# Moving one k and q step ahead of a decay step, and pairing two more head pairs, in a linear-attention and two-MLP kernel

## The reference

```python
for t in range(S):                      # 768 tokens, state is 48 x 48 for each batch and head
    state = alpha[:, :, t, :, None] * state + einsum('bhd,bhe->bhde', k[:, :, t], v[:, :, t])
    y[:, :, t] = einsum('bhd,bhde->bhe', q[:, :, t], state)
x = y as (batch * token, head * 48)
x = square(maximum(x @ w_in, 0)) @ w_out          # first MLP
out = silu(x @ w2_in) @ w2_out                    # second MLP
```

## Time and profile before

| what | value |
|---|---|
| median of 3 runs | 886.68 us (886.6 to 889.64) |
| the profiled execution's own time | 888.62 us |
| its span on the core | 887.0 us |
| PE busy | 862.5 us, 97% of the span |
| DVE busy | 544.8 us, 61% |
| ACT busy | 436.5 us, 49% |
| mean granted PE clock over the span | 0.99 |

### The profile page before, as it was taken

One profiled execution on the slowest core, in us unless ns is written; L12 is line 12 of the kernel. 1 busy time (PEld: TensorE's weight loads), 2 busy tenths in 40 slices (PEclk: granted clock), 3 DMA queues, 4 the chain that ended last, 5 costly groups with the idle time before them and its releaser, 6 DMA issues.

```text
span 887.0 us, 17687 instructions
## 1 busy us (share of the span) xinstructions
PE 862.5 (97%) x6834; PEld 714.2 (81%) x6834; DVE 544.8 (61%) x1090; ACT 436.5 (49%) x788; POOL 106.1 (12%) x127
## 2 busy tenths in 40 slices
PE   7999999998999899989999999999999999999998
PEld 6778788887778777878888888888888888888898
DVE  7789888877576657653234565555855446766620
ACT  5756654454445445534567654445543336545510
POOL 3463200000000000000165003002020003000000
PEclk9999999999999899989999999999999999999999
DMA  8884444334242414100321353000130000110010
GB/s 169 232 235 110 107 114 113 79 84 106 55 107 71 97 31 101 55 18 11 116 72 54 66 113 89 1 1 1 37 107 0 1 1 1 36 37 1 1 48 28
DMA packets 134204, 60.04 MB, mean 68 GB/s; under 512 B 81824, under 2 KB 129312, under 8 KB 134112
## 3 DMA queue, kind: packets, MB, share of 16 engines
q1 hardware_dynamic: 130800, 58.14, 26.6%
q10 hardware_dynamic: 3312, 0.69, 0.4%
HBM read 45.02 MB, written 9.44 MB: 61 GB/s over the span
## 4 chain that ended last, share of the span: by engine, by line
PE 83%; DVE 8%; issue 4%; ACT 3%; SPq 1%; DMA 1%; DVEq 0%; ACTq 0%
PE h_ps L1239 20%; PE z_ps L1210 17%; PE h_ps L1196 17%; PE z_ps L1275 11%; PE jobs L1275 7%; PE jobs L1295 3%; DVE decay L1784 3%; DVE decay L1769 2%; DVE kp L1738 2%; PE jobs L1062 1%; PE jobs L1073 1%; PE h_ps L1295 1%; ACT g L1507 1%; ACT g L1513 1%; DVE kp L1802 1%
## 5 line engine op out<-in xcount | busy, mean ns | idle before, releaser
L1507 ACT ACTIVATE g<-h_ps 128x512 f32<-128x512 f32 x96 | 57.1, 595 | 170.0 <-PE h_ps L1196 167.9
L1899 DVE TENSOR_TENSOR g_lo<-g,g_hi 128x512 fp32r<-128x512 f32 x96 | 68.1, 712 | 101.9 <-ACT g L1513 101.8
L1601 ACT ACTIVATE sum<-sum 128x512 f32<-128x512 f32 x96 | 60.6, 631 | 137.2 <-DVE sum L1960 112.2
L1960 DVE TENSOR_TENSOR sum<-h_ps,sum 128x512 f32<-128x512 f32 x120 | 82.9, 691 | 56.5 <-PE h_ps L1239 53.9
L1196 PE MATMUL h_ps<-x_hi,win_hi 128*128 128x512 f32 x288 | 114.1, 396 | 2.5 <-DVE x_lo L1891 0.9
L1210 PE MATMUL z_ps<-g_hi,wout_hi 128*128 128x512 f32 x282 | 115.4, 409 | 0.0
L1196 PE MATMUL h_ps<-x_lo,win_hi 128*128 128x512 f32 x288 | 112.3, 390 | 0.0
L1196 PE MATMUL h_ps<-x_hi,win_lo 128*128 128x512 f32 x288 | 112.2, 390 | 0.0
L1210 PE MATMUL z_ps<-g_hi,wout_lo 128*128 128x512 f32 x282 | 112.2, 398 | 0.0
L1210 PE MATMUL z_ps<-g_lo,wout_hi 128*128 128x512 f32 x282 | 111.9, 397 | 0.0
L1239 PE MATMUL h_ps<-s_hi,t_hi 128*128 128x512 f32 x264 | 103.1, 390 | 0.2 <-DVE sum L1960 0.2
(11 more groups left out here) (185 smaller groups left out, 1597.4 us busy)
## 6 DMA issues: line engine op xcount, KB each, us to landing
z_scratch<-z_sb SPq DMA_DIRECT2D x18, 256.0 KB, 2.7
pre<-z_scratch SPq DMA_DIRECT2D x18, 256.0 KB, 3.8
v_sb<-in_v SPq DMA_DIRECT2D x44, 96.0 KB, 2.5
out_x<-z_stage SPq DMA_DIRECT2D x80, 48.0 KB, 1.7
nat_a<-in_alpha SPq DMA_DIRECT2D x40, 88.0 KB, 2.3
nat_k<-in_k SPq DMA_DIRECT2D x40, 88.0 KB, 2.2
nat_q<-in_q SPq DMA_DIRECT2D x40, 88.0 KB, 2.3
nat_a<-in_alpha SPq DMA_DIRECT2D x40, 80.0 KB, 2.2
```

The costliest lines, as they stand in the source:

```text
L1507: nc.scalar.activation(g[f % 2][:], h_ps[f % 2][:], ACT.Relu).then_inc(act_made, 1)
L1601: nc.scalar.activation(at[:], at[:], ACT.Silu).then_inc(silu_made, 1)
L1899: nc.vector.tensor_tensor(low, g[f % 2][:], high.bitcast(F32), ALU.subtract).then_inc(g_lo_made, 1)
L1960: nc.vector.tensor_tensor(to[:], h_ps[(PRODUCTS * n + r) % 2][:], other[:], ALU.add).then_inc(summed, 1)
```

## The change

For the couples that go by the formula, KQ of the first pair moves from base - 1 to base - 2, which is the step of the second pair's A. In DVE's order within a step KQ comes before A. Pairs 4 and 5 become a couple, with steps of their own in the table. Pair 5 then uses the output tile `y_sb[0]`, as every coupled pair does, and its scores go into `y_sb[1]`; three waits follow this.

```diff
 def coupled(n):
-    return n >= COUPLED
+    return n >= COUPLED or n // 2 == PAIRS // 2
...
     if first < 14:
-        at = {8: {"A": 13, "KQ": 14, "S": 16, "I": 19, "Y": 20}, 9: {"A": 16, "KQ": 17, "S": 19, "I": 20, "Y": 22},
+        at = {4: {"A": 1, "KQ": 2, "S": 4, "I": 7, "Y": 8}, 5: {"A": 4, "KQ": 6, "S": 7, "I": 8, "Y": 10},
+              8: {"A": 13, "KQ": 14, "S": 16, "I": 19, "Y": 20}, 9: {"A": 16, "KQ": 17, "S": 19, "I": 20, "Y": 22},
...
     if n % 2 == 0:
-        return base + {"A": -4, "KQ": -1, "S": 0, "I": 3, "Y": outputs}[kind]
+        return base + {"A": -4, "KQ": -2, "S": 0, "I": 3, "Y": outputs}[kind]
...
             def y_copy(n):
                 y_slot_free(n // PAIRS, n % PAIRS)
-                if n > COUPLED:
+                if n > PAIRS and coupled(n - 1):
                     wait(act, y_moved[(n + 1) % 2], moved((n + 1) // PAIRS, (n + 1) % PAIRS))
...
             def a_turn(n):
-                if coupled(n):
+                if n > PAIRS + 1:
                     wait(dve, kt_made, n - 1)
...
             def s_stage(n):
-                wait(dve, y_made, n - 1 if n > COUPLED else n)
-                if n == COUPLED + 1:
+                wait(dve, y_made, n - 1 if coupled(n) and coupled(n - 1) else n)
+                if n in (PAIRS + 1, COUPLED + 1):
                     wait(dve, y_moved[n % 2], moved(n // PAIRS, n % PAIRS))
```

## The result

The changed kernel takes 875.46 us (median of 4 runs, 874.21 to 876.59), against 888.02 us for the kernel before on the same chips (4 runs, 886.6 to 889.64). The ratio is 0.9858, 95% interval 0.9829 to 0.9886. The profiled execution took 874.47 us with a span of 872.8 us, so 14.2 us less than the 887.0 us of before; 14.6 us were forecast.

The account below looks back on a forecast made before the run. PE was taken as the bound, nearly always busy, idling 12.0 us at the scores of five pairs. Waits 6.9, clock 7.4 and pairs 4 and 5 0.3 sum to 14.6 us: 888.62 to 874.0 us, range 867.5 to 880.0.

Parts of the forecast that it names:

- The scores' wait goes: PE's wait at the scores, 12.0 us over five couples, disappears because q is ready at about 203.8.
- It moves to the next first product: First products wait for the addition of Y, held by the later decay through ACT's queue: 1.6 or 0.9 us each.
- The gain of a couple is 2.61 us less d: d is the decay's delay on DVE; gains of 1.44 us three times and 1.27 us twice, 6.9 us in sum.
- The clock's 7.4 us: PE's lower clock behind waits at the scores cost 7.4 us by twin stretches; all of it counted as won.
- the rival with the falling clock: The clock still falls behind the remaining waits, so 3 to 7 us stay lost: 877 to 881.4 us; chance 0.15.
- Pairs 4 and 5, 0.3 us: Making pairs 4 and 5 a couple wins 0.2 to 0.5 us net, taken as 0.3 us.
- the rival of the costly second part: DVE adds pair 4's outputs late behind pair 6's decay, costing 2 to 4 us at worst: 877 us; chance 0.06.
- The median: The median of the runs was taken as 874.0 us, or 872.1 if 1.9 us are a fixed part of profiling.
- The claim that the spread goes: The 3 us by which runs of the kernel before differ should go where all waits are short.
- The stall did not go altogether: Rival: the output copy is not held by the sum of squares, no stall remains: 867.7 us; chance 0.12.
- The slower outcome: Rival: k and q find no idle time on DVE, d is 3.49 us: 892.7 us; chance 0.03.

Follow-up runs that it names:

- kernel with d = 3.49 us: The changed kernel with k and q of the first pair behind the low part, still ahead of the second pair's decay: 894.09 us, ratio 1.0044.
- kernel that keeps PE busy: The kernel before with 14 matmuls of 128x256 on PE ahead of the scores of pairs 14, 16, 18, 20 and 22: 881.36 us, ratio 0.9908.
- the first part alone: The kernel before with k and q of the first pair at base - 2 for five couples, pairs 4 and 5 single: 876.0 us, ratio 0.9837.
- all waits: The later-sum-of-squares kernel with the first pair's decay at base - 5 (couples 16, 20) and pair 4's output copy ahead of two weight copies: 867.94 us.

## Why the prediction was right, point by point

**The scores' wait goes.** Right: no wait at L1063, in all five couples. q was ready at 202.97 + 0.69 = 203.66 (203.8 forecast).

**It moves to the next first product and is held by the decay through ACT's queue.** Right, and shown rather than argued: with the sum of squares behind the copy all five waits went. The forecast waits were 1.6 us three times and 0.9 us twice; 1.37, 1.33 and 1.02 us, and 0.57 and 0.59 us, were seen. The starts were forecast better than the idle times, since an idle time is counted from the modelled end of the last matmul: product 37 came 7.89 us behind product 36, and 213.75 - 205.83 = 7.92 us was forecast.

**The gain of a couple is 2.61 us less d.** Right. Gains are counted here from first product base to base + 2. In the couples whose stretch had run at full clock before, the changed kernel gained 1.35 us (pair 14) and 1.24 us (pair 20), for 1.44 and 1.27 forecast. The term was 0.09 us too large for pair 14, because a first product that waits makes its next step 0.13 us longer (4.21 us; 4.09 in the kernel before, where product 37 did not wait). Couple 22 did not quite follow the pattern of 14, as the prediction has it: its wait was 2.49 us before and is 1.02 us now. The kernel with d = 3.49 us confirms the other side: its waits are 2.2 to 2.4 us longer.

**The clock's 7.4 us.** Right. Couples 16, 18 and 22 gained 2.84, 4.27 and 4.32 us; less the gain of their twins (1.24, 1.35, 1.35) this is 1.60, 2.92 and 2.97 us, against 1.61, 2.91 and 2.91. The kernel that keeps PE busy gave 7.41 us by the clock alone. The Trainium skill's way of pricing it, in "TensorE: Matmul & The Clock Gate", section "Terms", gave an estimate of 8.1 us, which was 0.7 us too high. Part of a half-clock stretch does not double: the 32 score matmuls took 0.69 us at full clock and 1.13 us at half clock (granted clock 0.50 from 296.28 to 298.00), which is 1.6 times as long.

```profile
296.28 1.13 PE L1062 MATMUL jobs<-qp,kp 48*64 48x64 f32 x32 [2.84 <-issue]
```

Of the waits that remain (1.37 us at most) none brought the clock down, and in the ten runs with k and q moved (four of the changed kernel, six of the first part alone) the mean clock is 0.999 or 1.00, so the rival with the falling clock is out for this kernel. The prediction had two reasons for this: the waits are shorter, and they lie between large matmuls. The second does not hold by itself, since waits of 2.8 to 3.7 us at the same place brought the clock down four times in five. There is some luck in the size: 7.4 us is what one execution lost, and the kernel before lost more or less from run to run.

**Pairs 4 and 5, 0.3 us.** Nothing that can be told from zero: counted from first product 0, product 36 stood 0.09 us earlier in the changed kernel, and 0.31 us later in the one with this part alone. The wait of first product 9 was forecast at 0.3 us and was 0.43 us, but its cause as forecast (two weight copies on ACT) was wrong. It is the decay of pair 6, which the rival of the costly second part named, at a smaller price. That the wait was forecast at about its size, from the wrong operations, is luck.

**The median.** 874.0 was forecast and 875.46 measured. The claim that the spread goes holds for the part that the clock made. On one chip 23 runs of the kernel before took 884.37 us (mean clock 0.996) to 896.58 us (0.983), and 6 runs of the first part alone 874.27 to 876.56 us. A spread of 2 us remains, which the prediction had not seen (last section); runs at its longer end lift the median over the sum.

**The rivals.** The stall did not go altogether, since the copy is held as said. The slower outcome needs d above 2.61 us: the kernel with k and q behind the low part has it, and took 894.09 us, 3.2 us more than the kernel before on its chip (892.7 us, or 4.1 us more, forecast).

## What to carry to other kernels

Before a late operation is moved ahead of another, ask who waits for that other one, and on which engine's queue: here moving k and q won 1.2 to 1.4 us of waits of 1.9 to 2.8 us, beside what the clock gave, and the rest needed an operation moved on another engine. Price a move by the idle time that it fills, not by the wait that it removes; the same move behind one more operation, where it fills none, made the kernel slower. A wait of PE can cost more than its length, where the clock falls behind it; filling it with matmuls that do nothing tells that share apart.

## What the runs showed of the hardware

The lower clock followed waits unevenly. In the kernel before it fell at the waits ahead of pairs 16, 18 and 22 (1.94, 2.84 and 2.49 us), and not at those of 14 and 20 (2.84 and 1.94 us). In the kernel with pairs 4 and 5 alone, whose waits are the same to 0.02 us, it fell at 14, 18 and 22. So the same wait of 2.84 us brought it in one execution and not in the other. Of waits of 2.8 to 3.7 us for the addition of Y four in five did, and none of the waits of first products of 1.4 us or less. The fall need not come at once: at pair 16 the clock was still 1.00 from 253.20 to 254.80, over the small matmuls behind the wait, and 0.50 from 255 to 257. The kernel before took from 884.37 to 896.58 us on one chip, with mean granted clocks from 0.996 to 0.983.

The end of the kernel has two lengths. In the changed kernel the last transfer, on ACT's queue, is sent at 870.76, and the span ends at 872.8:

```profile
870.76 0.38 ACTq L1691 DMA_DIRECT2D out_x<-z_stage  x1
```

In the kernel with the first part alone it is sent at 870.95, and the span ends at 874.7:

```profile
870.95 0.37 ACTq L1690 DMA_DIRECT2D out_x<-z_stage  x1
```

So 1.7 us more passed there behind the same instruction. By the profile's list of DMA issues, this transfer of 96 KB took 1.7 us from issue to landing in four of the eleven traces (before, changed, PE kept busy, all waits) and 3.1 to 3.9 us in the other seven, whatever the kernel. Four runs of the changed kernel have spans of 872.6, 872.8, 874.8 and 875.0 us, as two such ends would give; why the last transfer takes one or the other was not tried. The two medians of the kernel with the later sum of squares, 867.81 and 869.73 us, lie about as far apart.
